# Opening levels issued half by half, and a reordered turn between the two parts of a kernel

## The chip, the core and the metric

The kernel runs on one core of a Trainium2 chip. The metric is the device time of one execution in microseconds (us), the median of several runs. The core has a matrix engine (TensorE, PE in the profile), a vector engine (VectorE, DVE), an activation engine (ScalarE, ACT), a general engine (GpSimd, POOL) and queues for transfers (SyncE issues most of them, SPq; GpSimd issues some). Each engine works through its own instructions in order and waits on semaphores for the others.

## What is computed

The reference chains three blocks.

```
attention: per head, state S (48x48), for t in 768 steps:
    y_t = q_t S
    S   = S + beta_t k_t (v_t - S^T k_t)^T        (k_t normalised)
dense block:   x = (sigmoid(x Wg) * (x Wv)) Wo     (3072 tokens, 384 -> 1536 -> 384)
expert block:  expert = argmax of cosine(x, emb);  gate = its softmax share
               out = gate * relu(x W1[expert]) W2[expert]   (8 experts, 384 -> 1024 -> 384)
```

## The kernel before

The attention is worked in 24 groups of 128 time steps (8 heads each). A group needs the inverse of a triangular 128x128 matrix for each head. It is built in seven levels of doubling block size: the first comes from `first_inverse`, the six others (l = 1 to 6) each need a masked product (TensorE, L1231), a mask multiplied on (VectorE, L669), two products (TensorE, L1239 and L1242) and two casts from PSUM back to SBUF (ScalarE, L953 for `Xs`, L956 for `XTs`).

**Opening.** The first three groups (stages s = 0, 1, 2; `opening(s)` on each engine) run before the dense block has rows to work on. Here each level is done for heads 0 to 3 (half 0) and heads 4 to 7 (half 1), with semaphores of their own for each half. TensorE issues per level: `half_masked` for both halves, four filler matmuls (`warm`, 128x384, L1349, whose result nobody reads), `half_products` of half 0, one filler, `half_products` of half 1, two fillers. In places of the fillers stand other products of the stage (`expert_product` L1364, `state_update` L1307, `y_transposes` L1316, `key_transposes` L1167). VectorE computes the key norms of the next group (`norm_a`, `norm_b`, `norm_c`) ahead of the first mask. ScalarE casts `Xs` of both halves and then `XTs` of both, and casts the high parts of the dense weights between the levels (`weight_high`, L982 and L985); GpSimd subtracts their low parts (`weight_low`, L432 and L434). A stage ends with `half_residual` (L1250), `half_inverse` (L1257) and the products of the next group's keys (`gram`, L1194), which wait for the inverse.

**Main part.** From stage 3 on the levels of a group and the dense block's products (L1329, L1344) are interleaved on TensorE. In the last two steps, which have no group, VectorE also splits four of the eight pieces of expert 0's weights (`split_piece`: a cast L764 and a subtraction L769).

**Turn.** After the last dense product VectorE picks the experts of the last rows, counts them and computes the table of tiles: first the row of each tile's first token (`row_ok`, L911), for GpSimd, which loads the token numbers of a tile (`idt`) and gathers its rows (`xs`); then expert and slot of each tile (`tab_ok`, L921), for TensorE. Behind these come the gates of the last rows (`pay_ok`), a transpose of all gates on TensorE (L1548), their write to memory, and the rest of expert 0's weight pieces. TensorE runs 42 fillers, waits for `tab_ok`, runs 36, transposes the gates, runs 24, and then transposes the first gathered rows (L1555).

**Experts.** 31 tiles of 128 rows: `first_layer` (L1569, L1574), `second_layer` (L1585, L1589), with transposes between. SyncE loads experts 1 and 2 once the gates of tile 2 have been gathered. GpSimd subtracts low parts of the rows and of the hidden values (`rows_low`, `hidden_low`), and issues the scatter of finished tiles (`put`).

What stands in each engine's queue is written out by hand; nothing is scheduled by a planner.

Of the kernel before, what the change touches and what calls it, by code (L numbers as in the profile page):

```python
# [15 lines left out]
P = 128  # L16
# [5 lines left out]
E = 8  # L22
# [8 lines left out]
NT0 = 4  # L31
# [34 lines left out]
def build(nc, ctx, kv_d, qT_d, beta_d, betaT_d, mask_d, umask_d, lmask_d, emask_d, wg_d, wv_d, wo_d, emb_d, tau_d, w1_d, w2_d, woT_d, ids_d, rt_d, x2_d, reg_d, gate_d, out_d):  # L66
# [105 lines left out]
    tmp_te = sb("tmp_te", [P, NTP, E])  # L172
    tmp_e = sb("tmp_e", [P, E, NG])
# [221 lines left out]
    def _(pool):  # L395
# [118 lines left out]
        early = [pool.value_load(tint[0:1, 3, t:t + 1], min_val=0, max_val=REG - P) for t in range(NT0)]  # L514
        pool.wait_ge(scat, 16 * NG)

        def first_ids(t):
            pool.dma_start(idt[:, t, :], reg_d[bass.ds(early[t], P), 0:2]).then_inc(id_in[t], 16)
# [30 lines left out]
        for t in range(NT0):  # L549
            first_ids(t)  # L550
# [3 lines left out]
        gather(2)  # L554
        rows_low(0)
# [4 lines left out]
        for k in range(NT + 1):  # L560
            if k + 1 < NT:
                rows_low(k + 1)
            if k > 0:
                put(k - 1)
            if k < NT:
                hidden_low(k, 0)
                hidden_low(k, 1)
            if k + 4 < NT:
                load_ids(k + 4)
            if k + 3 < NT:  # L570
                gather(k + 3)
                gather_gates(k + 3)

    @block.vector
    def _(dve):
# [208 lines left out]
        def body(s):  # L784
# [12 lines left out]
            if routed(s - 1) is not None:  # L797
                place(routed(s - 1))
            if routed(s) is not None:
                rows_out(routed(s))  # L800
            if g is not None:
                level_mask(g, 1)
            if moe:
                gated(n + 1)
                if s > NG:
                    split_piece(2 * (s - NG - 1))
# [11 lines left out]
            if moe:  # L818
                gated(n + 2)
                if s > NG:  # L820
                    split_piece(2 * (s - NG - 1) + 1)
# [34 lines left out]
        def opening(s):  # L856
            cg = s - 1 if s > 0 else None
            gram_masks(s, 0)
            gram_masks(s, 1)
            norm_a(s + 1)  # L860
            norm_b(s + 1)
            norm_c(s + 1)
            for l in range(1, LEVELS):
                for hf in range(2):
                    half_mask(s, l, hf)
# [20 lines left out]
        gate_d(settled(NS - 1))  # L886
        wait(dve, out_ps, NF * NM)
# [12 lines left out]
        link(nc.vector.memset(rs[:, 2, :], 1.0))  # L900
        link(nc.vector.tensor_tensor_scan(rs[:, 3, :], rs[:, 2, :], rs[:, 1, :], 0.0, ALU.mult, ALU.add))
        link(nc.vector.tensor_tensor(rs[:, 4, :], rs[:, 3, :], rs[:, 1, :], ALU.subtract))
        link(nc.vector.scalar_tensor_tensor(rs[:, 5, :], rs[:, 4, :], float(-P), rt[:, RT_CAP:RT_CAP + E], ALU.mult, ALU.add))
        link(nc.vector.tensor_tensor(tmp_te[:, :, :], rs[:, 3, :].unsqueeze(1).to_broadcast([P, NTP, E]), rt[:, RT_TILE:RT_TILE + NTP].unsqueeze(2).to_broadcast([P, NTP, E]), ALU.is_le))
        link(nc.vector.tensor_reduce(tid[:, 0, :], tmp_te[:, :, :], AX.X, ALU.add))
        link(nc.vector.tensor_scalar(tid[:, 1, :], tid[:, 0, :], float(E - 1), None, ALU.min))
        link(nc.vector.tensor_tensor(tmp_te[:, :, :], tid[:, 1, :].unsqueeze(2).to_broadcast([P, NTP, E]), rt[:, RT_IOTA:RT_IOTA + E].unsqueeze(1).to_broadcast([P, NTP, E]), ALU.is_equal))
        link(nc.vector.tensor_tensor(tmp_te[:, :, :], tmp_te[:, :, :], rs[:, 5, :].unsqueeze(1).to_broadcast([P, NTP, E]), ALU.mult))
        link(nc.vector.tensor_reduce(tid[:, 4, :], tmp_te[:, :, :], AX.X, ALU.add))
        link(nc.vector.scalar_tensor_tensor(tid[:, 0, :], rt[:, RT_TILE:RT_TILE + NTP], float(P), tid[:, 4, :], ALU.mult, ALU.add))  # L910
        nc.vector.tensor_copy(tint[0:1, 3, :], tid[0:1, 0, :]).then_inc(row_ok, 1)  # L911
        dve.wait_ge(row_ok, 1)
        link(nc.vector.tensor_scalar(tid[:, 2, :], tid[:, 1, :], float(SLOTS), float(-SLOTS), ALU.is_ge, ALU.mult))
# [13 lines left out]
        for c in range(4, WC // PIECE):  # L927
# [5 lines left out]
    def _(act):  # L933
# [16 lines left out]
        def half_level(g, l):  # L950
# [3 lines left out]
            for hf in range(2):  # L954
# [205 lines left out]
    def _(pe):  # L1160
# [315 lines left out]
        def opening(s):  # L1476
# [15 lines left out]
            else:  # L1492
                expert_product(1)
                expert_product(2)
            first_inverse(s, 1)
# [5 lines left out]
            for l in range(1, LEVELS):  # L1501
                half_masked(s, l, 0)
                half_masked(s, l, 1)
# [6 lines left out]
                else:  # L1510
                    warm(4, pA)
                half_products(s, l, 0)
                warm(1, pC)
# [9 lines left out]
                else:  # L1523
                    warm(2, pC)
# [24 lines left out]
        warm(24)  # L1549
# [112 lines left out]
```

## Time and profile before

| what | value |
|---|---|
| median of 3 runs | 1221.64 us (1221.01 to 1223.2) |
| profiled execution | 1220.88 us, of which span 1219.2 us |
| PE busy | 1195.2 us (98%), 11615 matmuls |
| DVE busy | 690.5 us (57%) |
| ACT busy | 500.1 us (41%) |
| POOL busy | 581.0 us (48%) |
| granted TensorE clock | 0.999 |
| opening | 0 to 88.6 us |
| last dense product to first product of the experts | 892.6 to 913.4 us |

The span is the time from the first to the last instruction. Busy of PE counts the fillers. In the timeline, a row that merges several instructions gives their number after an x, and the time in brackets is what the engine stood idle before the row, with what released it. A matmul's shown duration overlaps the next one's, so distances are best read from start to start.

### The profile page before, as it was taken

What the parts mean: (1) busy time and instruction counts of PE and PEld (TensorE: products, weight loads), DVE (VectorE), ACT (ScalarE), POOL (GpSimd) and SP (SyncE); (2) the same over time, 40 slices, a digit from 0 to 9 for tenths busy, and PEclk for the clock granted to TensorE, in tenths of its full rate; (3) what the DMA queues carried; (4) which work ended last, traced back from release to release, by engine and by line L of the source; (5) the groups of instructions that cost most, each with busy time, mean ns of one, the idle gap of its engine ahead of it and who ended that gap; (6) DMA issues with size and microseconds to landing.
All of it is one profiled execution on the core that took longest, in us unless ns stands there. A gap on an engine that the chain in (4) does not pass through costs nothing.

```text
span 1219.2 us, 29378 instructions
## 1 busy us (share of the span) xinstructions
PE 1195.2 (98%) x11615; PEld 1094.9 (90%) x11615; DVE 690.5 (57%) x1541; ACT 500.1 (41%) x1143; POOL 581.0 (48%) x590
## 2 busy tenths in 40 slices
PE   6999999999999999999999999999989999999997
PEld 3779999999999999999999999999968899899996
DVE  5665566766566666656666666653474935555000
ACT  5654433343444334344433434442214444444443
POOL 6773334333343434324343432332337887777764
PEclk9999999999999999999999999999999999999999
DMA  6351011011101100110111011002016331443110
GB/s 224 110 173 30 24 41 30 30 30 31 37 28 35 30 30 30 30 42 24 34 30 33 27 29 36 9 22 89 30 34 233 139 125 60 154 166 109 44 39 1
DMA packets 48248, 74.77 MB, mean 61 GB/s; under 512 B 7797, under 2 KB 36789, under 8 KB 48116
## 3 DMA queue, kind: packets, MB, share of 16 engines
q1 hardware_dynamic: 41396, 61.82, 15.6%
q0 software_dynamic: 6720, 11.07, 2.9%
q8 instruction: 98, 1.61, 0.5%
q14 instruction: 34, 0.28, 0.1%
HBM read 61.59 MB, written 12.65 MB: 61 GB/s over the span
## 4 chain that ended last, share of the span: by engine, by line
PE 92%; DVE 5%; DMA 1%; issue 1%; POOL 1%; ACT 1%; SPq 0%; POOLq 0%; DVEq 0%; ACTq 0%
PE ps L1329 27%; PE ps L1344 13%; PE ps L1569 6%; PE ps L1585 6%; PE ps L1194 4%; PE ps L1574 3%; PE ps L1289 3%; PE ps L1589 3%; PE ps L1298 3%; PE ps L1219 3%; PE ps L1211 3%; PE ps L1222 2%; PE ps L1349 2%; PE ps L1599 2%; PE ps L1296 2%; PE ps L1266 2%
## 5 line engine op out<-in xcount | busy, mean ns | idle before, releaser
L440 POOL TENSOR_TENSOR gl<-sg,gh 128x256 fp32r<-128x256 f32 x144 | 108.8, 755 | 395.9 <-ACT gh L993 395.6
L1329 PE MATMUL ps<-xh,wgh 128*128 128x256 f32 x864 | 263.7, 305 | 0.0
L1329 PE MATMUL ps<-xl,wgh 128*128 128x256 f32 x864 | 243.4, 282 | 0.0
L1329 PE MATMUL ps<-xh,wgl 128*128 128x256 f32 x864 | 242.7, 281 | 0.0
L663 DVE TENSOR_TENSOR MP<-ps,mE 128x512 f16<-128x512 f32 x126 | 87.1, 691 | 157.8 <-PE ps L1211 155.9
L1329 PEld LDWEIGHTS ps<-xh,wgh 128*128 128x128 f32 x864 | 163.7, 189 | 7.9 <-issue 7.0
L1329 PEld LDWEIGHTS ps<-xl,wgh 128*128 128x128 f32 x864 | 164.3, 190 | 0.0
L1329 PEld LDWEIGHTS ps<-xh,wgl 128*128 128x128 f32 x864 | 163.6, 189 | 0.0
L989 ACT ACTIVATE sg<-ps 128x256 f32<-128x256 f32 x144 | 55.4, 385 | 262.0 <-PE ps L1329 262.0
L946 ACT CAST Xs<-ps 128x512 f16<-128x512 f32 x126 | 73.6, 584 | 137.8 <-PE ps L1219 137.8
L1344 PE MATMUL ps<-woh,gh 128*128 128x392 f32 x288 | 108.9, 378 | 1.2 <-POOL gl L440 1.2
L764 DVE CAST W<-W 128x768 fp32r<-128x768 f32 x64 | 55.0, 868 | 86.3 <-DMA W<-w_dram 86.3
L697 DVE TENSOR_TENSOR sg<-sg,ps 128x256 f32<-128x256 f32 x144 | 60.0, 416 | 71.7 <-ACT sg L989 70.0
L1344 PE MATMUL ps<-wol,gh 128*128 128x392 f32 x288 | 98.2, 341 | 0.0
L1344 PE MATMUL ps<-woh,gl 128*128 128x392 f32 x288 | 97.8, 340 | 0.0
L425 POOL TENSOR_TENSOR BA<-CT,BA 128x512 f32<-128x512 f16 x48 | 66.2, 1379 | 65.5 <-DVE CT L657 65.1
L1569 PE MATMUL ps<-W,xsh 128*128 x372 | 94.4, 402 | 1.2 <-issue 0.9
L1585 PE MATMUL ps<-W,hh 128*128 x496 | 93.6, 341 | 1.4 <-ACT hh L1136 1.4
L769 DVE TENSOR_TENSOR W<-W 128x768 fp32r<-128x768 f32 x64 | 87.9, 1381 | 0.3
L1585 PEld LDWEIGHTS ps<-W,hh 128*128 128x128 f32 x496 | 84.7, 188 | 1.7 <-issue 1.6
L1569 PEld LDWEIGHTS ps<-W,xsh 128*128 128x128 f32 x372 | 67.8, 189 | 15.7 <-issue 1.6
L541 POOL TENSOR_TENSOR hl<-hr,hh 128x512 fp32r<-128x512 f32 x62 | 80.6, 1337 | 0.2
(217 smaller groups left out, 2647.4 us busy)
## 6 DMA issues: line engine op xcount, KB each, us to landing
W<-w_dram SPq DMA_DIRECT2D x16, 1536.0 KB, 9.7
betaT<-betaT_dram SPq DMA_DIRECT2D x48, 128.0 KB, 3.0
kin<-kv_dram SPq DMA_DIRECT2D x24, 192.0 KB, 2.7
kqT<-qT_dram SPq DMA_DIRECT2D x48, 96.0 KB, 2.6
vin<-kv_dram SPq DMA_DIRECT2D x24, 192.0 KB, 2.3
x_dram<-x2r SPq DMA_DIRECT2D x24, 192.0 KB
woT<-woT_dram SPq DMA_DIRECT2D x1, 2304.0 KB, 8.5
stage<-w_gate_dram SPq DMA_DIRECT2D x6, 384.0 KB, 8.9
```

The costliest lines, as they stand in the source:

```text
L425: pool.tensor_tensor(BA[:, 0, hs, :], CT[:, hs, :], BA[:, 0, hs, :], ALU.add).then_inc(lof_ok, 1)
L440: pool.tensor_tensor(gl[n % 2][:, :], gp[n % 2][:, :], gh[n % 2][:, :].bitcast(F32), ALU.subtract).then_inc(gl_ok, 1)
L541: pool.tensor_tensor(hl[t % 2][:, hs, :], hr[:, hs, :], hh[t % 2][:, hs, :].bitcast(F32), ALU.subtract).then_inc(hl_ok, 1)
L663: nc.vector.tensor_tensor(cols(MP[l], l, 0), packed(pC, l), mE[:, l - 1, :].rearrange("p (a c) -> p a c", c=1 << l).unsqueeze(1).to_broadc ...
L697: nc.vector.tensor_tensor(gp[n % 2][:, :], sg[n % 2][:, :], ps[n % 2][:, TB:2 * TB], ALU.mult).then_inc(gp_ok, 1)
L769: ins = nc.vector.tensor_tensor(W12[:, e % SLOTS, 1, cs], W12[:, e % SLOTS, 1, cs].bitcast(F32), W12[:, e % SLOTS, 0, cs].bitcast(F32), AL ...
L946: nc.scalar.copy(cols(Xs, l, 0), packed(pA, l)).then_inc(xx_ok, 1)
L989: nc.scalar.activation(sg[n % 2][:, :], ps[n % 2][:, 0:TB], ACT.Sigmoid).then_inc(sg_ok, 1)
L1329: mm = pe.matmul(ps[n % 2][:, kind * TB:(kind + 1) * TB], w[:, kind, a, cs], v[m % 2][:, a, :], start=(a == 0 and x == 0), stop=(a == KT - ...
L1344: mm = pe.matmul(ps[2 + j][:, 0:ROW], g[n % 2][:, j * P:(j + 1) * P], w[:, f, :], start=(f == 0 and x == 0), stop=(f == NF - 1 and x == 2))
L1569: pe.matmul(ps[c][:, :], xsh[q][:, a, :], W12[:, bass.ds(s, 1), k, cs].rearrange("p o f -> p (o f)"), start=(a == 0 and k == 0), stop=False)
L1585: pe.matmul(ps[5 + r][:, 0:HD], hh[r][:, a, :], W12[:, bass.ds(sl, 1), k, cs].rearrange("p o f -> p (o f)"), start=(a == 0 and k == 0), st ...
```

## The change

**Opening.** On TensorE `half_masked` of half 1 moves behind `half_products` of half 0 in every level; half 0 of level 1 moves ahead of the second `first_inverse`. The fillers ahead of the first products go from four to three, those at a level's end from two to one. ScalarE casts `Xs` and `XTs` of half 0 and then both of half 1. VectorE does the mask of level 1, half 0, ahead of `norm_a`, and that of half 1 between `norm_a` and `norm_b`. The casts of the weights stay where they are on ScalarE.

**Turn.** The table of first rows needs one operation fewer of its own and no equality test, works on seven columns instead of eight, and a constant is set earlier; the sum and the minimum for the tile's expert move behind `row_ok`. GpSimd reads one row number ahead of the first load of `idt` instead of four, and loads those of tile 3 behind the first three gathers. The fillers behind the transpose of the gates go from 24 to 10. A fifth piece of expert 0's weights is split in the last step of the main part.

**Tail.** At the last tile but one, GpSimd's `put` moves behind both `hidden_low`.

```
@@ gpsimd
-        early = [pool.value_load(tint[0:1, 3, t:t + 1], ...) for t in range(NT0)]
+        first_row = pool.value_load(tint[0:1, 3, 0:1], min_val=0, max_val=REG - P)
...
-        for t in range(NT0):
-            first_ids(t)
+        pool.dma_start(idt[:, 0, :], reg_d[bass.ds(first_row, P), 0:2]).then_inc(id_in[0], 16)
+        load_ids(1)
+        load_ids(2)
         pool.wait_ge(x2_out, 32 * NM)
         gather(0)
         gather(1)
         gather(2)
+        load_ids(3)
         rows_low(0)
...
-            if k > 0:
+            if 0 < k and k != NT - 1:
                 put(k - 1)
             if k < NT:
                 hidden_low(k, 0)
                 hidden_low(k, 1)
+            if k == NT - 1:
+                put(k - 1)
@@ vector
+            if s == NS - 1:
+                split_piece(2)
...
-                    split_piece(2 * (s - NG - 1))
+                    split_piece(3 * (s - NG - 1))
...
+            half_mask(s, 1, 0)
             norm_a(s + 1)
+            half_mask(s, 1, 1)
             norm_b(s + 1)
             norm_c(s + 1)
             for l in range(1, LEVELS):
                 for hf in range(2):
-                    half_mask(s, l, hf)
+                    if l > 1:
+                        half_mask(s, l, hf)
...
-        link(nc.vector.tensor_tensor(rs[:, 4, :], rs[:, 3, :], rs[:, 1, :], ALU.subtract))
-        link(nc.vector.scalar_tensor_tensor(rs[:, 5, :], rs[:, 4, :], float(-P), rt[...], ALU.mult, ALU.add))
+        link(nc.vector.tensor_scalar(rs[:, 4, :], rs[:, 1, :], float(-P), float(CAP), ALU.mult, ALU.add))
...
-        for c in range(4, WC // PIECE):
+        for c in range(5, WC // PIECE):
@@ scalar
             for hf in range(2):
                 wait(act, half_xx_ps[hf], (LEVELS - 1) * g + l)
                 nc.scalar.copy(half_cols(Xs, hf, l, 0), ...)
-            for hf in range(2):
                 wait(act, half_xts_ps[hf], (LEVELS - 1) * g + l)
                 nc.scalar.copy(half_cols(XTs, hf, l, 1), ...)
@@ tensor
+            half_masked(s, 1, 0)
             first_inverse(s, 1)
...
             for l in range(1, LEVELS):
-                half_masked(s, l, 0)
-                half_masked(s, l, 1)
+                if l > 1:
+                    half_masked(s, l, 0)
...
-                    warm(4, pA)
+                    warm(3, pA)
                 half_products(s, l, 0)
+                half_masked(s, l, 1)
                 warm(1, pC)
                 half_products(s, l, 1)
...
-                    warm(2, pC)
+                    warm(1, pC)
...
-        warm(24)
+        warm(10)
```

The next two lists are TensorE's, level 2 of the second opening stage: L1231 (before) and L1234 (changed) are the masked products, L1349/L1352 the fillers, L1239/L1242 and L1242/L1245 the products; semaphores with a 2 in their names are those of half 1. Before:

```order
L1231 MATMUL ps<-Xs,CT 128x64 [waits xx_ok]
L1231 MATMUL ps<-Xs,CT 128x64 x3
L1231 MATMUL ps<-Xs,CT 128x64 [waits xx2_ok]
L1231 MATMUL ps<-Xs,CT 128x64 x3
L1349 MATMUL ps<-mE,mI 128x384 x4
L1239 MATMUL ps<-MP,XTs 128x64 [waits xts_ok,mp_ok]
L1239 MATMUL ps<-MP,XTs 128x64 x3
L1242 MATMUL ps<-XTs,MP 128x64 x4
L1349 MATMUL ps<-mE,mI 128x384
L1239 MATMUL ps<-MP,XTs 128x64 [waits xts2_ok,mp2_ok]
L1239 MATMUL ps<-MP,XTs 128x64 x3
L1242 MATMUL ps<-XTs,MP 128x64 x4
```

Changed:

```order
L1234 MATMUL ps<-Xs,CT 128x64 [waits xx_ok]
L1234 MATMUL ps<-Xs,CT 128x64 x3
L1352 MATMUL ps<-mE,mI 128x384 x3
L1242 MATMUL ps<-MP,XTs 128x64 [waits xts_ok,mp_ok]
L1242 MATMUL ps<-MP,XTs 128x64 x3
L1245 MATMUL ps<-XTs,MP 128x64 x4
L1234 MATMUL ps<-Xs,CT 128x64 [waits xx2_ok]
L1234 MATMUL ps<-Xs,CT 128x64 x3
L1352 MATMUL ps<-mE,mI 128x384
L1242 MATMUL ps<-MP,XTs 128x64 [waits xts2_ok,mp2_ok]
L1242 MATMUL ps<-MP,XTs 128x64 x3
L1245 MATMUL ps<-XTs,MP 128x64 x4
```

The masked product of half 1 (waits xx2_ok) stood right behind that of half 0; it now stands behind half 0's products, and only one filler lies between it and half 1's products, which wait for its mask (mp2_ok).

The next two lists are VectorE's, second opening stage: L606/L604 end the norms before, L669 (changed: L670) is a mask, L596 and L585 to L587 are `norm_a`, L590 begins `norm_b`. Before:

```order
L590 SCALAR_TENSOR_TENSOR quo<-n,inv 128x8 [waits rd]
L591 SCALAR_TENSOR_TENSOR gs<-gs,quo 128x8 [waits rd]
L604 TENSOR_SCALAR quo<-gs 128x8 [waits rd]
L606 RECIPROCAL rn<-quo 128x8 [waits kn_ok,rd]
L669 TENSOR_TENSOR MP<-ps,mE 128x128x2 [waits m_ps]
L669 TENSOR_TENSOR MP<-ps,mE 128x128x2 [waits m2_ps]
L669 TENSOR_TENSOR MP<-ps,mE 128x64x4 [waits m_ps]
```

Changed:

```order
L660 TENSOR_TENSOR XTs<-CT,mL 128x512 [waits ct_ok]
L670 TENSOR_TENSOR MP<-ps,mE 128x128x2 [waits m_ps]
L596 TENSOR_REDUCE n<-kn 128x8 [waits sq_ok]
L585 TENSOR_SCALAR n<-n 128x8 [waits n2_ok]
L586 TENSOR_SCALAR gs<-n 128x8 [waits rd]
L587 TENSOR_SCALAR gs<-gs 128x8 [waits rd]
L670 TENSOR_TENSOR MP<-ps,mE 128x128x2 [waits m2_ps,rd]
L590 RECIPROCAL inv<-gs 128x8
```

Both masks of level 1 stood behind all of the norms; they now stand around `norm_a`, and the rest of the norms lies ahead of level 2.

The next two lists are GpSimd's in the turn: `tint` is the table of first rows, `idt` the token numbers of a tile. Before:

```order
L514 TENSOR_LOAD tint [waits row_ok]
L514 ISA x2
L514 TENSOR_LOAD tint
L514 ISA x2
L514 TENSOR_LOAD tint
L514 ISA x2
L514 TENSOR_LOAD tint
L514 ISA x2
L518 ISA [waits scat]
L518 DMA idt<-reg_dram 128x2
L518 ISA
L518 DMA idt<-reg_dram 128x2
```

Changed:

```order
L514 TENSOR_LOAD tint [waits row_ok]
L514 ISA x2
L546 ISA [waits scat]
L546 DMA idt<-reg_dram 128x2
L520 TENSOR_LOAD tint
L520 ISA x2
L521 ISA
L521 DMA idt<-reg_dram 128x2
L520 TENSOR_LOAD tint
L520 ISA x2
L521 ISA
L521 DMA idt<-reg_dram 128x2
```

Three of the four reads of the table moved behind the first load of token numbers.

## Rows read from the trace of the kernel before

**Rows 1.** Timeline, TensorE, second opening stage (columns: start, us, engine, line, operation, idle before).
```profile
51.70 0.28 PE L1239 MATMUL ps<-MP,XTs 128*128 128x64 f16 x4
...
51.94 0.33 PE L1349 MATMUL ps<-mE,mI 128*128 128x384 f16 x1
...
52.67 0.47 PE L1231 MATMUL ps<-Xs,CT 128*128 128x64 f16 x8
...
52.98 0.81 PE L1349 MATMUL ps<-mE,mI 128*128 128x384 f16 x4
...
53.63 0.28 PE L1239 MATMUL ps<-MP,XTs 128*128 128x64 f16 x4
```

**Rows 2.** Timeline, same stage: masks, first product of level 1, casts.
```profile
49.13 0.70 DVE L669 TENSOR_TENSOR MP<-ps,mE 128x256 f16<-128x256 f32 x2
...
49.56 0.29 PE L1239 MATMUL ps<-MP,XTs 128*128 128x64 f16 x4 [0.93 <-DVE MP L669]
...
52.98 0.76 DVE L669 TENSOR_TENSOR MP<-ps,mE 128x256 f16<-128x256 f32 x2 [0.47 <-PE ps L1231]
...
53.94 0.77 ACT L953 CAST Xs<-ps 128x256 f16<-128x256 f32 x2 [0.60 <-PE ps L1239]
```

**Rows 3.** Timeline, same stage: first residual product, which ends the levels.
```profile
60.94 0.22 PE L1250 MATMUL ps<-Xs,CT 128*128 128x128 f16 x1
```

**Rows 4.** Timeline, VectorE, same stage: first and last step of the key norms.
```profile
46.33 0.55 DVE L595 TENSOR_REDUCE n<-kn 128x8 f32<-128x384 f32 x1
...
49.02 0.20 DVE L606 RECIPROCAL rn<-quo 128x8 f32<-128x8 f32 x1
```

**Rows 5.** Timeline, TensorE, first opening stage.
```profile
22.22 0.29 PE L1239 MATMUL ps<-MP,XTs 128*128 128x64 f16 x4
...
24.26 1.02 PE L1364 MATMUL ps<-woT,enT 128*8 128x512 f32 x2
...
35.54 0.22 PE L1250 MATMUL ps<-Xs,CT 128*128 128x128 f16 x1
```

**Rows 6.** Timeline, VectorE and GpSimd, starts of stages two and three.
```profile
41.20 1.82 POOL L432 TENSOR_TENSOR wgl<-stage,wgh 128x768 fp32r<-128x768 f32 x1
...
41.64 1.93 DVE L657 TENSOR_TENSOR CT<-mNI,BA 128x512 f16<-128x512 f16 x1
...
65.45 1.82 POOL L434 TENSOR_TENSOR wol<-stage,woh 128x768 fp32r<-128x768 f32 x1
...
67.03 0.79 DVE L657 TENSOR_TENSOR CT<-mNI,BA 128x512 f16<-128x512 f16 x1
```

**Rows 7.** Busy time by stretch (PE first), granted clock before the DMA share.
```profile
15.00:20.00 5.00, 3.67 (x15) 0.94 (x16) 4.83 (x9) 1.79 (x3) 1.80 (x1) 1.00 1.03 392
```

**Rows 8.** Timeline, VectorE, last step but one of the main part.
```profile
876.45 0.42 DVE L697 TENSOR_TENSOR sg<-sg,ps 128x256 f32<-128x256 f32 x1 [2.30 <-ACT sg L989]
```

**Rows 9.** Timeline, VectorE, tables of the turn.
```profile
897.01 0.17 DVE L903 SCALAR_TENSOR_TENSOR rs<-rs,rt 128x8 f32<-128x8 f32 x1
...
898.38 0.42 DVE L907 TENSOR_TENSOR tmp_te<-tid,rt 128x256 f32<-128x256 f32 x1
...
899.97 0.17 DVE L911 CAST tint<-tid 1x32 int32<-1x32 f32 x1
```

**Rows 10.** Timeline, TensorE, the turn.
```profile
902.11 6.02 PE L1349 MATMUL ps<-mE,mI 128*128 128x384 f16 x36 [0.91 <-DVE tint L921]
...
912.09 0.49 PE L1555 MATMUL ps<-mI,xs 128*128 128x128 f32 x3
```

**Rows 11.** Timeline, GpSimd, the turn.
```profile
903.44 2.29 POOL L518 DMA_DIRECT2D idt<-reg_dram  x4 [5.26 <-issue]
...
906.44 1.17 POOL L532 DMA_INDIRECT xs<-x_dram,idt  x1 [0.71 <-issue]
```

**Rows 12.** Waits of TensorE from 905 us to the end (total, times, longest).
```profile
PE ps L1569 <- DVE W L769: 0.3, 1, 0.3
```

**Rows 13.** Timeline, TensorE, the last tile.
```profile
1212.06 1.55 PE L1589 MATMUL ps<-W,hl 128*128 x8
```

More of the change, by code:

```diff
@@ L30 @@
 SLOTS = 3
-NT0 = 4
 WC1 = KT * F2
@@ L172, in build @@
     tmp_te = sb("tmp_te", [P, NTP, E])
+    tmp_row = sb("tmp_row", [P, NTP, E - 1])
     tmp_e = sb("tmp_e", [P, E, NG])
@@ L513, in _ @@
         pool.wait_ge(row_ok, 1)
-        early = [pool.value_load(tint[0:1, 3, t:t + 1], min_val=0, max_val=REG - P) for t in range(NT0)]
+        first_row = pool.value_load(tint[0:1, 3, 0:1], min_val=0, max_val=REG - P)
         pool.wait_ge(scat, 16 * NG)
-        def first_ids(t):
-            pool.dma_start(idt[:, t, :], reg_d[bass.ds(early[t], P), 0:2]).then_inc(id_in[t], 16)
         def load_ids(t):
@@ L820, in body @@
                 if s > NG:
-                    split_piece(2 * (s - NG - 1) + 1)
+                    split_piece(3 * (s - NG - 1) + 1)
             if g is not None:
@@ L886, in _ @@
         gate_d(settled(NS - 1))
+        link(nc.vector.memset(rs[:, 2, :], 1.0))
         wait(dve, out_ps, NF * NM)
@@ L899, in _ @@
         link(nc.vector.tensor_reduce(rs[:, 1, :], tmp_e[:, :, :], AX.X, ALU.add))
-        link(nc.vector.memset(rs[:, 2, :], 1.0))
         link(nc.vector.tensor_tensor_scan(rs[:, 3, :], rs[:, 2, :], rs[:, 1, :], 0.0, ALU.mult, ALU.add))
-        link(nc.vector.tensor_tensor(rs[:, 4, :], rs[:, 3, :], rs[:, 1, :], ALU.subtract))
-        link(nc.vector.scalar_tensor_tensor(rs[:, 5, :], rs[:, 4, :], float(-P), rt[:, RT_CAP:RT_CAP + E], ALU.mult, ALU.add))
+        link(nc.vector.tensor_scalar(rs[:, 4, :], rs[:, 1, :], float(-P), float(CAP), ALU.mult, ALU.add))
         link(nc.vector.tensor_tensor(tmp_te[:, :, :], rs[:, 3, :].unsqueeze(1).to_broadcast([P, NTP, E]), rt[:, RT_TILE:RT_TILE + NTP].unsqueeze(2).to_broadcast([P, NTP, E]), ALU.is_le))
[L905 to L909, printed above, removed]
+        link(nc.vector.tensor_tensor(tmp_row[:, :, :], tmp_te[:, :, 0:E - 1], rs[:, 4, 0:E - 1].unsqueeze(1).to_broadcast([P, NTP, E - 1]), ALU.mult))
+        link(nc.vector.tensor_reduce(tid[:, 4, :], tmp_row[:, :, :], AX.X, ALU.add))
         link(nc.vector.scalar_tensor_tensor(tid[:, 0, :], rt[:, RT_TILE:RT_TILE + NTP], float(P), tid[:, 4, :], ALU.mult, ALU.add))
@@ L912, in _ @@
         dve.wait_ge(row_ok, 1)
+        link(nc.vector.tensor_reduce(tid[:, 0, :], tmp_te[:, :, :], AX.X, ALU.add))
+        link(nc.vector.tensor_scalar(tid[:, 1, :], tid[:, 0, :], float(E - 1), None, ALU.min))
         link(nc.vector.tensor_scalar(tid[:, 2, :], tid[:, 1, :], float(SLOTS), float(-SLOTS), ALU.is_ge, ALU.mult))
```

## The prediction

> **What bounds the kernel now.** I read the chain of waits first, then the timeline of each engine where the change puts its hands: the opening, the last step of the main part, the turn, the last tile. Between 93 and 889 us nothing is moved, so three places count.
>
> In the opening the reader should look at TensorE from start to start. One level of the second stage runs from 51.70 to 53.63, 1.93 us, and is full: half 0's products 0.24, a filler 0.16 (four take 0.65), half 1's products 0.24, two fillers 0.33, both masked products 0.31, four fillers 0.65 [rows 1]. Nearly as long is the chain behind it. From the masked product to the start of its mask on VectorE 0.31 (52.67 to 52.98), and from a mask's start to its product 0.43 (49.13 to 49.56): 0.74 from masked product to product [rows 1, 2]. From product to the cast on ScalarE is another 0.31 (53.63 to 53.94) [rows 1, 2]. Because both halves' masked products stand together, the masks run back to back and the 0.74 is paid once per level. Ahead of the first level stand the key norms, 46.33 to 49.22 [rows 4]; TensorE waits 0.93 us for the mask behind them [rows 2].
>
> In the turn TensorE waits 0.91 us for the table (`tab_ok`), then runs 36 fillers; the first gathered rows are transposed at 912.09 with no idle time ahead of them [rows 10]. So it is TensorE's own list of fillers that ends last there, not the gather. From 905 us to the end it then waits only 0.3 us for weights [rows 12]: in the expert part a microsecond gained at the turn is a microsecond of the kernel, if the loads move with it.
>
> **Opening, the levels.** Changed, half 1's masked product stands behind half 0's products. In one level TensorE now goes: masked product 0, wait, products 0, masked product 1, wait, products 1, one filler. The 0.74 is exposed twice, since the three fillers (0.49) and the one (0.16) are shorter than it. Sum: 2 x (0.74 + 0.24) + 0.16 = 2.12 us against 1.93 [rows 1, 2]. The fillers taken out buy nothing; what was filler becomes waiting.
>
> From half 0's products of level 2 to the residual product the second stage takes 60.94 - 51.70 = 9.24 us [rows 1, 3]. Changed: four levels of 2.12, about 0.2 more where the transposes of y stand in for one filler, and 0.24 + 0.74 + 0.24 + 0.32 = 1.54 behind level 6: 10.2, so +1.0. The same for the third stage. ScalarE's new order (both casts of half 0, then of half 1) is costed at nothing: half 1's cast is wanted only 0.98 us after half 0's product, and the weight casts, which in the old order delayed level 5 and 6 by a few tenths, fall into the waits. Bounds for the cost of one level: from -0.35 (no wait left, fillers alone: 1.93 less two of them and nothing else gets late) to +0.4 (the casts late as well). I take +0.19, since all its terms are rows of the same kind.
>
> **Opening, ahead of the levels.** The mask of level 1, half 0, no longer waits for the norms. In the second stage TensorE reaches its products at about 48.1: it stood idle 0.93 before 49.56, and one filler and two masked products leave the stretch ahead [rows 2]. Half 1's masked product follows 0.24 later and its mask at 48.65; behind that VectorE has the rest of the norms, 1.7 of their 2.9 us [rows 4] (the start of them, 1.1, now fits into a wait). So the first mask of level 2 comes at 50.7 and its products at 51.15 instead of 51.70 [rows 1]: -0.55. What goes as a wait for level 1 comes back as one for level 2. In the third stage TensorE's own list stands closer behind, and I get -0.2. Bounds: 0 and -1.5 (all that level 1 gains).
>
> **Opening, first stage.** It has products of the expert embedding as fillers, 0.96 each (two in 1.02, overlapping) [rows 5]. Two levels become 0.24 + 0.74 + 0.24 + 0.96 + 0.13 + 0.96 = 3.27, two are 2.12, one is 2.79 with the expert transposes in it, and 1.54 at the end: 15.1 us against 35.54 - 22.22 = 13.3 [rows 5], +1.8; level 1 itself starts 0.4 earlier, since its mask does not wait for norms that a weight subtraction holds up. Net +1.4.
>
> **Opening, the shared port.** In the second stage VectorE's subtraction CT, started at 41.64 under a weight subtraction of GpSimd (41.20 to 43.02), took 1.93 us; in the third, started at 67.03 just before the end of one (65.45 to 67.27), 0.79 [rows 6]. The norms now end 1.4 us later against their stage, and GpSimd's weight subtractions hang on them. That of 65.45 would move by 1.4 for the norms and 1.4 for the first stage, to 68.2 to 70.0, while CT moves by 1.9 to 68.9: it would be caught for up to 1.2 us. Bounds 0 and 1.2; I take 0.3, because the start of GpSimd's chain can shift either way. The Trainium skill (SBUF — State Buffer, Who interferes with whom) says that a VectorE instruction with two SBUF inputs contends with a GpSimd instruction that reads SBUF, one with a single SBUF input doesn't. By that rule the masks that are moved (PSUM and one SBUF input) are never caught; the trace agrees, two took 0.76 together at 52.98 [rows 2]. The rule leaves CT as the one to watch.
>
> Opening: 1.4 + (1.0 - 0.55) + (1.0 - 0.2) + 0.3 = +2.95 us.
>
> **Last step of the main part.** The fifth piece costs VectorE some 1.5 us between two gated products; it stands idle 2.30 us there [rows 8]. Zero, and 0.2 if the cover is short.
>
> **Turn.** Up to `tab_ok` VectorE loses a small step (0.17 and 0.03 between) [rows 9], an equality test (0.42 and 0.03) [rows 9], a memset (0.1), and an eighth of two long steps (0.07 together): 0.82. TensorE's 36 fillers start that much earlier, since it waited 0.91 for them [rows 10]. Fourteen fillers fewer at 0.1625 are 2.28. The first transposes move from 912.09 to 909.0, -3.1, if the rows have arrived.
>
> They should: `row_ok` (899.97, plus 0.17) [rows 9] comes earlier by 0.82, a sum (0.45) and a minimum (0.2), 1.47 in all. Between it and the first load of token numbers at 903.44 stood four reads of the table, 3.3 us or 0.8 each [rows 11]; three of them now stand behind it, two ahead of the first gather. The first load comes at about 900.3 and the gather between 902.9 and 904.1 instead of 906.44 [rows 11]. Before, the rows were there at the latest 5.65 after the gather's start (912.09 - 906.44) [rows 10, 11]; even with all of that they are there by 909.7, 0.7 late at worst. The load of tile 3's numbers (0.6 plus a read) is over before the first row subtraction is wanted at 910.5. The write of the gates, their gathers and with them the loads of experts 1 and 2 also move by 3.0 to 3.1, so the one wait of 0.3 us in the expert part stays as it is [rows 12]. Bounds -2.3 and -3.4; I take -3.1.
>
> **Tail.** The last group of products starts at 1212.06 with no idle time ahead [rows 13], so it did not wait for the subtraction that `put` leaves the way to: zero.
>
> **Sum.** 1220.88 + 2.95 - 3.1 = 1220.7 for the profiled execution. That execution lies 0.76 under the median of the runs, so the forecast for the median is 1221.5.
>
> **Rivals.** Half by half is a gain after all (chance 0.2). If the levels keep 1.93 us, because a mask's way is shorter when its half comes alone or because ScalarE was the true bound in levels 4 to 6, what stays is the earlier start: -0.4, -0.55 and -0.2. With the turn that is -4.2, 1217.4. For it: TensorE is seen waiting for a cast ahead of later levels' products, and the stage's fillers shrink by more than the level grows. Against it: TensorE's order leaves nothing between masked product and product that is as long as 0.74.
>
> The gain of the turn is not there, because the gather or the weights end last (0.1): -3.1 becomes -1, 1223.6. For it: four DMAs and two reads lie ahead of the gather. Against: the rows had 5.65 us and need not have taken them.
>
> Slower: TensorE's clock falls in the opening (0.1). It now stands idle some 0.5 us of each level. At 1.2 GHz fillers, products and masked products take twice as long: a level is 0.26 + 0.98 + 0.48 + 0.74 + 0.13 + 0.48 + 0.33 = 3.4 instead of 2.12, 1.3 more; a stage of six such levels costs 7.7 and the kernel comes to 1229. It decides from two to three such levels on. Against it: from 15 to 20 us TensorE was busy 3.67 of 5 us, as it would be now, and the granted clock stayed 1.00 [rows 7].
>
> **How the numbers follow.** The forecast (gain of the turn eaten by the opening) has 0.6. Its own range: opening +1.5 to +4.5, turn -3.4 to -2.5, so 1219.6 to 1223.5. About 2.4 us (0.2%) is what a measurement of this kernel can tell from no change. Faster by more: the first rival, and a small part of the forecast: 0.23. Slower by more: the clock and the far end of port and missing turn: 0.13. Same: 0.64. The range that holds 8 in 10 reaches down towards the first rival and up over the second: 1217.8 to 1223.8.
>
> **What would show it.** Right: levels of 2.1 us in stages two and three and two waits for masks in each; the main part starting 2 to 4 us later (`gram` of stage 3 after 90.5 instead of 88.6); `row_ok` 1.5 and `tab_ok` 0.8 earlier against the last dense product; first expert products 3.1 us nearer to it, no new wait behind. Wrong: levels of under 1.95, or transposes of the first rows that wait for the gather, or a granted clock below 1.

## The result, and the profile after

| kernel | median of the runs | lowest to highest | profiled execution, span |
|---|---|---|---|
| before | 1221.64 us (9 runs) | 1220.98 to 1223.2 | 1220.88, 1219.2 |
| changed | 1225.76 us (9 runs) | 1224.74 to 1228.58 | 1224.91, 1223.2 |

The ratio is 1.0033 with a 95% interval of 1.0023 to 1.0042: slower by 0.33%, 4.1 us. The forecast was 1221.5 and the range ended at 1223.8.

Where the 4 us are, read from start to start (us after the start of the span; a stage begins with `gram`):

| stretch | before | after | difference |
|---|---|---|---|
| start to the first stage's products of level 1 | 22.22 | 23.31 | +1.1 |
| from there to `gram` of stage two (at 39.11; 43.73) | 16.89 | 20.42 | +3.5 |
| stage two (to 64.50; 69.95) | 25.39 | 26.22 | +0.8 |
| stage three (to 88.56; 95.50) | 24.06 | 25.55 | +1.5 |
| last `x2r` (VectorE's copy of the last dense rows out of PSUM) to the experts' first product | 20.81 | 17.73 | -3.1 |
| the rest | | | +0.1 |

The turn gave what was forecast. The opening cost 7.0 us and not 2.95, and 1.6 of the 7.0 lie ahead of everything that was changed (last section). Without them the edits of the opening cost 5.3.

First TensorE, two levels of the second stage after the change; it answers to [rows 1]:

```profile
57.03 0.28 PE L1234 MATMUL ps<-Xs,CT 128*128 128x64 f16 x4
57.15 0.65 PE L1352 MATMUL ps<-mE,mI 128*128 128x384 f16 x3
57.83 0.29 PE L1242 MATMUL ps<-MP,XTs 128*128 128x64 f16 x4
...
58.08 0.28 PE L1234 MATMUL ps<-Xs,CT 128*128 128x64 f16 x4
58.19 0.33 PE L1352 MATMUL ps<-mE,mI 128*128 128x384 f16 x1
58.87 0.29 PE L1242 MATMUL ps<-MP,XTs 128*128 128x64 f16 x4 [0.35 <-DVE MP L670]
...
60.28 0.29 PE L1242 MATMUL ps<-MP,XTs 128*128 128x64 f16 x4
...
62.52 0.29 PE L1242 MATMUL ps<-MP,XTs 128*128 128x64 f16 x4
```

A level is now 62.52 - 60.28 = 2.24 us (57.83 to 60.28 has transposes of y in it). From a masked product to its products it takes 0.80 for half 0 (57.03 to 57.83) and 0.79 for half 1 (58.08 to 58.87). So 2.24 is 0.80 + 0.25 + 0.79 + 0.25 and one filler, 0.16: nothing else is in it. The view of TensorE's waits from 0 to 100 us says the same in one line; after:

```profile
PE ps L1242 <- DVE MP L670: 7.5, 20, 0.5
```

Before, the line of that pair read:

```profile
PE ps L1239 <- DVE MP L669: 1.6, 2, 0.9
```

Two waits, of 0.93 and 0.67 (the norms, [rows 2]), became twenty of at most 0.5. That is about one per level and not the two that the prediction named as a sign: ahead of half 0's products the last filler's shown duration reaches to the product (57.15 + 0.65 = 57.80), so the profile counts no wait there, though from start to start 0.19 us of it is waiting.

Why 0.80 and not 0.74 is in VectorE's rows of the same stage, which answer to [rows 2]:

```profile
55.14 0.37 DVE L670 TENSOR_TENSOR MP<-ps,mE 128x256 f16<-128x256 f32 x1
...
57.35 0.42 DVE L670 TENSOR_TENSOR MP<-ps,mE 128x256 f16<-128x256 f32 x1 [0.17 <-PE ps L1234]
...
58.39 0.42 DVE L670 TENSOR_TENSOR MP<-ps,mE 128x256 f16<-128x256 f32 x1 [0.62 <-PE ps L1234]
```

The first stands right behind another instruction and takes 0.37; TensorE's products follow 0.43 after its start (55.57). The others start out of idle time and take 0.42; the products follow after 0.48. The pair of [rows 2] from which 0.43 was read stood right behind the norms, which end at 49.22 [rows 4].

In the first stage the way is longer still, and the fillers there are products of the expert embedding (TensorE, after; answers to [rows 5]):

```profile
23.31 0.29 PE L1242 MATMUL ps<-MP,XTs 128*128 128x64 f16 x4
...
29.58 1.02 PE L1367 MATMUL ps<-woT,enT 128*8 128x512 f32 x2
30.54 0.29 PE L1242 MATMUL ps<-MP,XTs 128*128 128x64 f16 x4
...
30.78 0.28 PE L1234 MATMUL ps<-Xs,CT 128*128 128x64 f16 x4
30.90 0.33 PE L1352 MATMUL ps<-mE,mI 128*128 128x384 f16 x1
31.66 0.29 PE L1242 MATMUL ps<-MP,XTs 128*128 128x64 f16 x4 [0.43 <-DVE MP L670]
...
32.93 0.29 PE L1242 MATMUL ps<-MP,XTs 128*128 128x64 f16 x4
```

30.78 to 31.66 is 0.88, and the level is 32.93 - 30.54 = 2.39 us. The longer way was there before the change. From the masked product to its mask it took 0.40 in this stage, against the 0.31 of the second stage:

```profile
26.92 0.41 PE L1231 MATMUL ps<-Xs,CT 128*128 128x64 f16 x8
...
27.32 0.95 DVE L669 TENSOR_TENSOR MP<-ps,mE 128x256 f16<-128x256 f32 x2 [2.24 <-PE ps L1231]
```

Why it is longer there is open.

The turn after the change, all three engines; it answers to [rows 9 to 11]:

```profile
899.63 0.24 DVE L898 COPY x2r<-ps 128x8 f32<-128x8 f32 x2 [1.31 <-issue]
...
905.46 0.17 DVE L913 CAST tint<-tid 1x32 int32<-1x32 f32 x1
...
907.29 0.59 POOL L546 DMA_DIRECT2D idt<-reg_dram  x1 [2.11 <-DMA reg_dram<-pay,slot]
...
908.11 0.16 DVE L925 CAST tint<-rs 1x8 int32<-1x8 f32 x1
...
910.43 1.01 POOL L529 DMA_INDIRECT xs<-x_dram,idt  x1 [0.30 <-issue]
...
916.03 0.49 PE L1560 MATMUL ps<-mI,xs 128*128 128x128 f32 x3
...
917.36 1.93 PE L1574 MATMUL ps<-W,xsh 128*128 x7
```

Against the last `x2r` (892.61 before, 899.63 now) `row_ok` moved from 7.36 to 5.83, `tab_ok` from 9.28 to 8.48, the gather from 13.83 to 10.80, the first transposes from 19.48 to 16.40, the first product from 20.81 to 17.73. TensorE stands idle ahead of neither of the last two. The first load of token numbers is now released, by the profile, by the write to `reg_dram` that it reads, 2.11 us, and no longer by the reads of the table. The waits of TensorE from 905 us to the end show no new one; its wait for a weight piece is the 0.3 of [rows 12] under the new line numbers:

```profile
PE ps L1574 <- DVE W L770: 0.3, 1, 0.3
```

### The profile page after: what moved, and what is told of

It is laid out like the page before. It is cut to its first block, busy times and chain, and to the rows that moved or that the text cites. A ratio compares the mean times of both kernels' runs of the same rounds, so it can differ in the third digit from the quotient of the medians.

```text
span 1223.2 us, 29305 instructions
## 1 busy us (share of the span) xinstructions
PE 1196.6 (98%) x11578; PEld 1092.1 (89%) x11578; DVE 695.0 (57%) x1539; ACT 499.9 (41%) x1143; POOL 579.5 (47%) x590
## 4 chain that ended last, share of the span: by engine, by line
PE 92%; DVE 4%; DMA 1%; issue 1%; POOL 1%; ACT 1%; SPq 0%; POOLq 0%; DVEq 0%; ACTq 0%
PE ps L1332 27%; PE ps L1347 13%; PE ps L1574 6%; PE ps L1590 6%; PE ps L1197 4%; PE ps L1292 3%; PE ps L1301 3%; PE ps L1579 3%; PE ps L1594 3%; PE ps L1222 3%; PE ps L1214 3%; PE ps L1225 2%; PE ps L1352 2%; PE ps L1604 2%; PE ps L1299 2%; PE ps L1269 2%
```

## The experiments

Each was run beside the kernel before on the same chip; a ratio is to those runs. "The turn alone" is the changed kernel with the opening of before.

### The two halves of the change: `open_only` and `turn_only`

Edit of the first: the opening's part of the diff on the kernel before. Edit of the second, the reverse on the changed kernel, on all three engines:

```
@@ tensor
-            half_masked(s, 1, 0)
             first_inverse(s, 1)
...
-                if l > 1:
-                    half_masked(s, l, 0)
+                half_masked(s, l, 0)
+                half_masked(s, l, 1)
...
-                    warm(3, pA)
+                    warm(4, pA)
                 half_products(s, l, 0)
-                half_masked(s, l, 1)
...
-                    warm(1, pC)
+                    warm(2, pC)
@@ vector, scalar: as before
```

> The kernel before with only the opening's edits (all three engines); turn, weight pieces and tail as before. Theory A (the levels pay the way from masked product to product twice; all of the loss is in the opening and all of the gain in the turn): about 7 us slower than before, 1228 to 1229, the first product of the main part's keys at 95 to 96 us, expert part unchanged. Theory B (the turn's edits cost something of their own, so that the 3.1 us seen there are lost elsewhere): as the changed kernel, +4 us. Theory C (the slow first 18 us of the changed kernel's profile, fillers 0.34 us each instead of 0.2, is chance and not the change): the start here is fast in some profiles and slow in others; with a fast start about +5.5 us.

> The changed kernel with the opening of before on all three engines; turn, fifth weight piece and tail changed. Theory A: 3.1 us faster than before, about 1218.5, opening as long as before (main part's first key product at 88.6 us). Theory B: no faster than before. Theory C: start as in before or slow, whichever chance gives.

Measured: 1228.54 us for the opening alone, ratio 1.0056 (1.0042 to 1.007), and 1219.32 for the turn alone, ratio 0.9975 (0.9965 to 0.9985). The turn alone beats both kernels. The opening's stretches are those of the changed kernel (20.42, 26.22, 25.54), and with the turn alone those of before (16.89, 25.37, 24.05): the two halves do not touch each other. Theory A is right on the place of the loss. Its figure of about 7 us held the slow start of the changed kernel's profile, and that `open_only` came near it is in part chance: its profiled execution (1229.38) began fast, but the wait for a transfer was 1.3 us longer than before, the clock fell behind it (last section), and level 1 starts 3.1 us later than its edits account for. Theory C's 5.5 us with a fast start is what the stretches give.

### Which engine's order costs: `pe_old`, `dve_old`, `act_old`, `act_only`, `dve_only`

The first three are the changed kernel with one engine's order in the opening as before; the last two are the turn alone with one engine's new order. TensorE's edit is the one above, the others are

```
@@ scalar (act_old; act_only has the reverse)
                 nc.scalar.copy(half_cols(Xs, hf, l, 0), ...)
+            for hf in range(2):
                 wait(act, half_xts_ps[hf], (LEVELS - 1) * g + l)
@@ vector (dve_old; dve_only has the reverse)
-            half_mask(s, 1, 0)
             norm_a(s + 1)
-            half_mask(s, 1, 1)
             norm_b(s + 1)
             norm_c(s + 1)
...
-                    if l > 1:
-                        half_mask(s, l, hf)
+                    half_mask(s, l, hf)
```

> The changed kernel with TensorE's order and fillers of the opening restored; VectorE still does half 0's first mask ahead of the norms, ScalarE still casts half by half. Theory A (TensorE's order is what costs): levels of about 1.95 us again, the loss of 4 us gone and about 1218 to 1219.5. Rival (VectorE's norms behind the first masks are what costs, since they hold up level 2 and, through the norms, GpSimd): stays within 1.5 us of the changed kernel.

> The changed kernel with only VectorE's order of the opening restored: all norms ahead of both first masks. Theory A: levels stay at 2.25 us, level 1 starts 1.5 us later in each stage and level 2 0.5 us later: slower than the changed kernel by 0.5 to 1.5 us, 1226.5 to 1227.5. Rival (the norms' place is what costs): faster than the changed kernel by 2 us or more.

> The changed kernel with only ScalarE's order of the opening restored (Xs of both halves, then XTs of both). Theory A: half 0's XTs is then cast behind half 1's Xs, about 2.1 us after half 0's products, just before the next level's products want it at 2.25: level 2.25 to 2.35, time within 1 us of the changed kernel. Rival (ScalarE's order is what costs): levels under 2.1 us and 2 us or more faster than the changed kernel.

> The changed kernel with TensorE's and VectorE's opening of before, and only ScalarE casting half by half. With both masked products side by side on TensorE, half 1's Xs now comes one cast (0.27 us) later, and half 1's masked product, mask and products with it. Theory A: levels of 1.93 grow to at most 2.1, the opening by 1 to 2.5 us over the version with the turn alone (ratio 0.9975): 1220 to 1221.5. Rival (harmless, ScalarE has slack): same as the turn alone, 1218.5 to 1219.3.

> The kernel with the turn alone changed, and VectorE's new order in the opening besides (both masks of level 1 around norm_a, norm_b and norm_c behind them); TensorE keeps both masked products together and its old number of fillers. It tells how the 3.6 us are to be split by which TensorE's old order in the changed kernel (1223.4, VectorE and ScalarE new) lay above the turn alone (1219.3); ScalarE's new order alone was 0.4. Theory A (the norms, moved behind level 1, hold up the masks of level 2, and TensorE's old order gets no more out of the earlier start because half 1's masked product already stands ahead of the products): 1222 to 1223, the start of gram of the last opening stage about 3 us later than with the turn alone, and level 1 to level 2 in the stages two and three some 1 us longer. Theory B (the two orders, VectorE's and ScalarE's, only cost together): 1219.3 to 1220.0, the same within 0.5 us as the turn alone. Both allow a profile with the slow start of the clock, which adds 1.6 us ahead of the first level and nothing between the stages.

| kernel | new order on | median us, ratio (interval) | first stage, two, three |
|---|---|---|---|
| `turn_only` | none | 1219.32, 0.9975 (0.9965 to 0.9985) | 16.9, 25.4, 24.1 |
| `act_only` | ScalarE | 1219.71, 0.9977 (0.9968 to 0.9986) | 17.1, 25.4, 24.1 |
| `dve_only` | VectorE | 1225.52, 1.0033 (1.0022 to 1.0043) | 17.6, 26.2, 26.0 |
| `pe_old` | VectorE, ScalarE | 1223.39, 1.0009 (0.9999 to 1.002) | 17.8, 26.1, 26.0 |
| `dve_old` | TensorE, ScalarE | 1227.6, 1.0045 (1.0031 to 1.0059) | 20.4, 28.4, 26.1 |
| `act_old` | TensorE, VectorE | 1225.84, 1.0029 (1.0017 to 1.004) | 20.4, 26.5, 25.5 |
| changed | all three | 1225.76, 1.0033 (1.0023 to 1.0042) | 20.4, 26.2, 25.6 |

The stretches (us) come from one execution each, the first from the products of level 1. The 28.4 holds a fall of the clock (last section). `pe_old` met neither of its forecasts (1218 to 1219.5, or within 1.5 us of the changed kernel): of the 5.9 us that the changed kernel's stretches lie above those of `turn_only`, 3.6 stay with VectorE's order. `dve_old` came out 0.1 above theory A's range, and `act_only` between its two.

ScalarE's order is worth at most 0.3 us either way (`act_only` 0.2 in the first stage, `act_old` 0.3 in the second). TensorE's order makes the first stage 20.4 with either order of VectorE, 3.5 over before: there its levels are the cost. VectorE's order alone costs 3.5 us in the stretches (0.7, 0.8, 2.0), and theory A of the last expectation named the wrong way for most of it. (Its profiled execution, 1222.08, is its fastest run; the median lies 3.4 above, with a granted clock down to 0.993. No trace of such a run was kept, so the 3.5 rest on the stretches alone.) VectorE and GpSimd in `dve_only`, start of stage three:

```profile
68.36 1.14 DVE L658 TENSOR_TENSOR CT<-mNI,BA 128x512 f16<-128x512 f16 x1
...
68.92 2.25 POOL L434 TENSOR_TENSOR wol<-stage,woh 128x768 fp32r<-128x768 f32 x1
...
69.53 1.91 DVE L660 TENSOR_TENSOR XTs<-CT,mL 128x512 f16<-128x512 f16 x1
```

and in `turn_only`, the same place:

```profile
68.44 0.77 DVE L658 TENSOR_TENSOR CT<-mNI,BA 128x512 f16<-128x512 f16 x1
...
69.25 0.43 DVE L660 TENSOR_TENSOR XTs<-CT,mL 128x512 f16<-128x512 f16 x1
```

Two VectorE instructions with both inputs in SBUF take 3.05 us instead of 1.20, +1.85, while GpSimd works beside them, and GpSimd's own subtraction takes 2.25 instead of 1.82. The norms end later, GpSimd's `kn` waits for them, and its weight subtractions slide into the next stage's start. `pe_old` has the same rows (0.99 and 1.91 there). The Trainium skill (SBUF — State Buffer, Who interferes with whom), which the prediction weighed, says that a VectorE instruction with two SBUF inputs contends with a GpSimd instruction that reads SBUF and one with a single SBUF input does not; these rows agree. The prediction named `CT` alone as the one to watch; `XTs`, whose inputs `CT` and `mL` both lie in SBUF, is hit harder here. What theory A did name, level 1 to level 2 longer (79.22 - 75.89 = 3.33 against 2.13), is given back by the earlier level 1 in stage three; in the first stage it stays as the 0.7.

With TensorE's new order as well, the same slide hits less. VectorE and GpSimd of the changed kernel, a subtraction of stage two and the start of stage three:

```profile
56.09 1.81 POOL L432 TENSOR_TENSOR wgl<-stage,wgh 128x768 fp32r<-128x768 f32 x1
...
71.44 1.82 POOL L434 TENSOR_TENSOR wol<-stage,woh 128x768 fp32r<-128x768 f32 x1
...
72.48 1.32 DVE L658 TENSOR_TENSOR CT<-mNI,BA 128x512 f16<-128x512 f16 x1
```

The 1.32 is 0.55 over the same row of `turn_only`. The mask at 57.35 (shown above), with one input in PSUM, lies wholly under the subtraction of 56.09 and keeps the 0.42 of the others. So the engines' costs do not add: over `turn_only` the stretches are 3.5 longer for VectorE alone, 8.6 for TensorE with ScalarE (`dve_old`, a fall of the clock in it) and 5.9 for all three, with two different mechanisms.

### Is the mask's way exposed, whatever TensorE does meanwhile: `fill_wait`

```
                 else:
-                    warm(3, pA)
+                    warm(4, pA)
                 half_products(s, l, 0)
                 half_masked(s, l, 1)
-                warm(1, pC)
+                warm(4, pC)
                 half_products(s, l, 1)
```

> The changed kernel with fillers put into the two waits of a level: four instead of three ahead of half 0's products (0.65 us), four instead of one ahead of half 1's (0.65 us), both shorter than the 0.79 us from a masked product to its products. Theory A (both ways are exposed, whatever TensorE does in them): levels stay at 2.25 us in stages two and three, the best executions stay at 1224.7, although 72 fillers are added (12 us of TensorE work). Rider: if the executions of the changed kernel above 1226 are those in which the idle time let the clock fall within the opening, they are gone here, and the median falls to 1224 to 1225. Rival (TensorE's own list bounds the level, as it did before): each level grows by 0.65 us, 18 levels, +11 us.

Measured: 1225.63 us, ratio 1.0028 (1.0018 to 1.0038). TensorE, stage three, one level:

```profile
80.41 0.28 PE L1234 MATMUL ps<-Xs,CT 128*128 128x64 f16 x4
80.53 0.81 PE L1352 MATMUL ps<-mE,mI 128*128 128x384 f16 x4
81.21 0.29 PE L1242 MATMUL ps<-MP,XTs 128*128 128x64 f16 x4
```

Four more fillers in a level and the level is as long as before them: half 1's way is 0.80 (80.41 to 81.21), filled or idle. The exposure is shown. (The stages two and three are 0.16 longer each; that is the fourth filler ahead of level 1's products, where TensorE's own list ends last.) The fastest run, 1223.33, lies 1.4 below the 1224.7 that was expected: this kernel's profile began fast (last section). TensorE's waits for masks are gone from the list of waits, the time is not. That fillers would spare the runs above 1226 us turned out wrong: they are still there.

### Taking the exposure away: `skew`

Half 1's products of a level move behind half 0's masked product of the next level:

```
                 if l > 1:
                     half_masked(s, l, 0)
+                    warm(1, pA)
+                    half_products(s, l - 1, 1)
...
-                    warm(3, pA)
+                    warm(2, pA)
                 half_products(s, l, 0)
                 half_masked(s, l, 1)
                 warm(1, pC)
-                half_products(s, l, 1)
...
-                    warm(1, pC)
+                    warm(2, pC)
-            warm(1, pC)
+            half_products(s, LEVELS - 1, 1)
```

> The changed kernel with TensorE's order of the opening altered again: half 1's products of level l - 1 are issued behind half 0's masked product of level l, so that each half's mask is made while the other half's products and masked product run. Same matmuls; two fillers and one ahead of half 0's products, one behind half 1's masked product, two at a level's end. Theory A (the order on TensorE costs 0.3 us a level because each way is waited out alone): level falls to 1.6 to 1.9 us, opening at least as short as before, total 1216 to 1219, faster than the kernel before by 3 to 5 us. Rival (a half's way has lengthened for another reason, ScalarE's or VectorE's order): levels stay at 2.1 us or more and the time over 1222.

Measured: 1222.77 us, ratio 1.0004 (0.9991 to 1.0017), 3 us under the changed kernel and 4 above the upper end of theory A (1216 to 1219), whose level was right and whose time was not: the stretches are 18.1, 26.5 and 25.4, so the gain lies in the first stage, and the other two stay as long as in the changed kernel. A level without disturbance falls to 1.69 (57.83 to 59.52), below the old 1.93. But TensorE now runs into ScalarE's queue (ScalarE and TensorE, stage two):

```profile
60.18 0.85 ACT L985 CAST wgh<-stage 128x768 fp32r<-128x768 f32 x1
60.92 0.40 ACT L957 CAST Xs<-ps 128x256 f16<-128x256 f32 x1
...
61.37 0.29 PE L1234 MATMUL ps<-Xs,CT 128*128 128x64 f16 x4 [0.85 <-ACT Xs L957]
```

`Xs` stands behind a cast of weights of 0.85 us, and TensorE waits as long. One level shows that half by half can be shorter than the pair if each half covers the other's way. That a whole opening can, with ScalarE's weight casts elsewhere, is not shown; it was not tried.

### Does TensorE's filler list still end the turn: `turn_warm2`

```
-        warm(10)
+        warm(2)
```

on the turn alone.

> The kernel with the turn alone changed, and the ten fillers between the transpose of the gates and the transposes of the first rows cut to two (8 x 0.1625 = 1.3 us less). Theory A (TensorE's own list of fillers is still what ends last there): the first transposes come 1.3 us nearer to the last dense product, the same holds for the experts' first product unless VectorE's weight pieces or the rows end later, and the kernel falls by 1.0 to 1.3 us, to 1218.0 to 1218.3. Theory B (the gathered rows, whose gather began 6.95 us before the transposes, or the weight pieces, whose last subtraction ended 0.7 us before them, now end last): TensorE waits for one of them ahead of the transposes or of the first product, and the gain is 0 to 0.7 us, 1218.6 to 1219.3. Theory C (the loads of experts 1 and 2 hang on the gates and do not move, so a wait for weights appears later in the expert part that takes the gain back): the first product is earlier by 1.3, a wait for the weights of expert 1 or 2 grows by as much, and the time stays at 1219.3.

Measured: 1217.93 us, ratio 0.997 (0.996 to 0.998), the fastest kernel of the study. Its span (1215.7) is 3.5 us shorter than that of before. TensorE and VectorE:

```profile
907.86 0.49 PE L1556 MATMUL ps<-mI,xs 128*128 128x128 f32 x3
...
908.85 0.96 DVE L770 TENSOR_TENSOR W<-W 128x768 fp32r<-128x768 f32 x1
...
909.96 3.07 PE L1570 MATMUL ps<-W,xsh 128*128 x12 [0.47 <-DVE W L770]
```

The transposes come 15.16 us after `x2r` (892.70) instead of 16.40, but the first product 17.26 instead of 17.73: it now waits 0.47 for the last weight piece. Of 1.3 us of fillers 0.5 are gained, theory B. The lowest runs of the two kernels, 1217.39 and 1217.95, lie 0.56 apart, as the wait says. The medians lie 1.4 apart; the 0.9 beyond the half microsecond go with the clock (last section), not the edit.

## Why the prediction was wrong

**The turn** was right in every step that it priced: 3.08 us against 3.1, `row_ok` 1.53 and `tab_ok` 0.80 earlier against 1.47 and 0.82. That the first load would wait for the write to `reg_dram` was not in it and cost nothing. The bound was TensorE's own list, and `turn_only` shows it alone.

**What failed is the term "The 0.74 is exposed twice", 2 x (0.74 + 0.24) + 0.16 = 2.12.** The mechanism was right, as `fill_wait` shows; the size was not. The way from masked product to products is 0.80 in the stages two and three and 0.88 in the first. 0.05 of the difference is that the 0.43 was read from a mask right behind other work, while the masks in question start out of idle time. Levels two to six cost +1.58 in stage two and three each, not +1.0 (half 0's products of level 2 to `gram`: 12.80 to 14.38 and 12.62 to 14.20). The way stands nine times in such a stretch, twice in each of four levels and once behind the last: nine times 0.06 are most of the 0.6.

**First stage: +1.4 forecast (+1.8 and -0.4), about +3.0 found** (+3.53 in the levels, -0.54 ahead of them, from the first group's `first_inverse` on). Each of its levels came out 0.3 longer than the sum (2.39 for 2.12, 3.6 for 3.27, 3.17 for 2.79). The sum for this stage took its 0.74 from rows of another; the same stage had rows to read it from (26.92 to 27.32 from masked product to mask, 0.40 and not 0.31). The way stands nine times here too, once only in the two levels where a product of the embedding covers half 0's: nine times 0.14 are 1.3. The rest are gaps of 0.1, five times, ahead of the embedding's products and transposes (25.76 to 25.98 for a masked product put at 0.13), which the sum left out. This is the largest miss, 1.7 of the 2.4 us.

**Ahead of level 2, stages two and three**: -0.75 and -0.09 from `gram` to the products of level 2, forecast -0.55 and -0.2. The second holds the port's +0.55.

**Port**: +0.55 against +0.3, at the place named, for the reason named. That without TensorE's new order it would be 1.85 was not seen.

**ScalarE's order at nothing**: right within 0.3 (`act_old`, `act_only`).

**Last step of the main part and tail at zero**: nothing in the rest of the span speaks against it (+0.1).

**Rivals.** Half by half as a gain is dead in this form: its price is the exposure, and only `skew` takes that away. The turn was not late. The clock rival is partly true in a way that was not forecast: TensorE did not slow in the profiled stages of the changed kernel, but in some executions of its relatives it did.

**What is left.** 5.3 - 3.1 is +2.2, and the profiled executions differ by 4.0, of which 1.6 is the slow start, which the prediction had nowhere. The medians differ by 4.1; the lowest runs of `fill_wait` and `act_old`, kernels with the same levels, are 1223.33 and 1223.46, about +2.4 over the lowest of before (1220.98). That +2.4 is the change. The other 1.7 of the median is not explained by its edits. The four fastest runs of the changed kernel lie at 1224.74 to 1224.98 with a granted clock of 0.999; the profiled one, with its slow start, is among them, and that the other three began so too is not shown. The other five lie at 1225.76 to 1228.58 with 0.995 to 0.997. Whether the emptier levels bring such runs about was not settled: `fill_wait` filled them and kept such runs. Less 1.6 us the median would be about 1224.1, still just outside the range, so chance made the miss larger and the sum made it a miss.

## What to carry to other kernels

When two halves share a round trip between engines, issuing them together pays the trip once, issuing them one behind the other pays it twice unless each half's work covers the other's trip; count the trips left uncovered, and multiply them by the number of levels, before counting how much earlier something starts. Read the trip's length from an instruction that starts as the one in question will, out of idle time or not, and in the same stage. And look at which engine's later end moves another's big instructions: here late norms moved GpSimd's subtractions under VectorE's, and VectorE's new order alone cost 1.85 us in a stage by that.

## What was not expected of the hardware

**A slow start of TensorE by chance.** TensorE's second group of fillers, in the changed kernel:

```profile
9.82 1.17 PE L1352 MATMUL ps<-mE,mI 128*128 128x384 f16 x3
...
15.61 1.78 PE L1352 MATMUL ps<-mE,mI 128*128 128x384 f16 x5
```

and in `turn_warm2`, with the same instructions up to there:

```profile
9.43 0.65 PE L1350 MATMUL ps<-mE,mI 128*128 128x384 f16 x3
...
13.64 0.99 PE L1350 MATMUL ps<-mE,mI 128*128 128x384 f16 x5
```

Matmuls at half rate (1.2 GHz for 2.4 GHz) from 9.8 to about 18 us put everything behind them 1.6 us later. Of the twelve profiled executions, those of the changed kernel, `turn_only` and `pe_old` started so, and `act_only` for its first group of fillers alone. TensorE's instructions up to there are the same in all, and kernels with the new opening (`open_only`, `dve_old`, `act_old`, `fill_wait`, `skew`) started fast, which speaks against the edits as the cause. The granted clock reads 1.00 in these stretches either way; only the duration of a known matmul shows it.

**Falls later on.** The table of busy times has TensorE's granted clock ahead of the DMA share. `dve_old`, second stage, behind a wait of 1.32 us for a mask:

```profile
53.00:57.00 4.00, 3.77 (x55) 2.67 (x56) 0.85 (x2) 1.29 (x4) 3.92 (x4) 0.57 0.76 204
```

Its three fillers take 1.06 there instead of 0.65, and the stage 28.4 us. `open_only`, behind a wait of 3.02 us for a DMA (before, TensorE waited 1.70 there and the clock stayed):

```profile
17.00:22.00 5.00, 4.18 (x10) 0.72 (x10) 0.70 (x2) 1.32 (x2) 1.80 (x1) 0.73 1.06 344
```

And `turn_only` in the turn, behind 1.63 us of idle time; before and the changed kernel stood idle 1.58 and 1.63 at that place and kept 1.00:

```profile
895.00:903.00 8.00, 7.36 (x37) 4.04 (x38) 6.69 (x32) 1.36 (x5) 2.61 (x4) 0.79 0.15 53
```

Its first fillers come at twice the distance, and the first product of the experts stands 19.13 us behind `x2r` instead of 17.73. That and its slow start are 3.0 us of its profiled 1220.7, and explain why the profile of `turn_warm2`, which had neither, looks better than its edit is. The profiled executions of `dve_old` and `fill_wait` have the same 19.13 in the turn. What decides whether the clock falls behind such a wait is open.
